# Causal masks added into the key bias by GpSimd, two runs of score products joined, and an order of transposes and copies to go with it

## The chip, the cores and the metric

The kernel runs on one core of a Trainium2 chip (trn2). The metric is the time of one execution on the device in microseconds (us), lower is better. The kernel before took 1081.54 us, the median of 3 runs (1081.49 to 1081.89).

## What is computed

Three layers in a row: causal attention with a decay bias, a mixture of 8 experts, and a product of two linear maps. Only the attention matters for the change:

```python
def _attn_ref(q, k, v, s):              # q, k, v: (2, 8, 576, 64); s: (2, 8, 576)
    scores = scale * np.matmul(q, k.transpose(0, 1, 3, 2))
    causal = np.triu(np.ones((S, S), dtype=bool), k=1)
    cum = np.cumsum(np.maximum(s, 0.0), axis=-1)
    bias = -(cum[:, :, :, None] - cum[:, :, None, :])
    scores = np.where(causal, -1000000000.0, scores + np.minimum(bias, 0.0))
    scores = scores - np.max(scores, axis=-1, keepdims=True)
    attn = np.exp(scores)
    attn = attn / (np.sum(attn, axis=-1, keepdims=True) + 1e-09)
    return np.matmul(attn, v)
```

Behind it come x @ w1[e], a ReLU and @ w2[e] for the experts, weighted by a gate of 8 Sinkhorn rounds, and (x @ w_a) * (x @ w_b) @ w_out. All is fp32 on the outside; the kernel splits fp32 numbers into a high and a low fp32r part and makes three products of each.

## The kernel before, in words

The attention takes the first 10% of the time. Its 16 heads go in 8 pairs. A loop over k from -1 to 8, written out by hand on each engine, is a software pipeline: in period k the scores of pair k are made while the probabilities of pair k-1 are transposed and multiplied with v, and pair k-2 is scaled into x. S_k below is the moment at which TensorE begins period k, with the tail transposes of pair k (line 1626). Within one pair, 576 query tokens are four tiles of 128 (t = 0 to 3) and a tail of 64 of both heads; tile t needs keys 0 to 128(t+1).

The order of TensorE in a period (lines 1813 to 1840): transpose_qk(k, 2), score(k, 0) with tiles 0 and 1, transpose_p(k-1, 5), the masks of tiles 0 and 1, transpose_p 2, score(k, 1) with tile 2, transpose_p 7, mask of tile 2, transpose_p 1, transpose_qk(k+1, 0), transpose_p 4, transpose_qk(k+1, 1), score(k, 2) with tile 3, transpose_p 3, mask, transpose_p 6, score_tail(k, 0), transpose_p 0, score_tail(k, 1) with its mask, spread_recips(k-1, 1) and (k-1, 0), attend(k-1, 1) and (k-1, 0). The score products (line 1662) use 64 rows of the array for each head, two heads side by side; all else uses 128 rows. A causal mask is a bf16 product of an identity with a triangle of large negative numbers, added into the same PSUM bank (lines 1671 and 1706): 8 of 128 columns and 1 of 64 for each pair.

VectorE adds the key bias to the scores while it reads them from PSUM and keeps the row minimum (biased, line 1179, biased_tail, line 1194; semaphore sc_done, 10 steps a pair), splits q and k (low_qk, 1157, 1160), copies some of the transposed probabilities out of PSUM (copy_pT, 1220), and makes the reciprocals of the row sums (invert, 1212). ScalarE makes the exponentials (exp_tile, 820; exp_tail, 830) and the other copies (798). The transposed probabilities go through a ring of two PSUM banks, so each transpose_p waits until the unit two places before it was copied.

GpSimd in period k (lines 706 to 724): spread_tail_queries(k) (630), wide_reciprocals(k-1) (641 and 644; TensorE's spread_recips(k-1) waits for them on rec_wide), low_x(k-2) (653), and in some periods work on the first expert weights.

The key bias is a row of cumulative sums, broadcast by DMA from DRAM to 128 partitions. SyncE issues all these loads in one queue, in program order. load_bias(p) (line 517) waits for sc_done of the tail of pair p-2, then issues two loads of 256 KB (line 523) and two of 144 KB for the tail (line 526); load_v and load_qk follow. In the kernel before only VectorE waits for them, at the first biased of pair p.

## Time and profile before

| | |
|---|---|
| median of 3 runs | 1081.54 us (1081.49 to 1081.89) |
| profiled execution | 1081.88 us, of which its span is 1080.1 us |
| TensorE busy | 1073.8 us (99%) |
| VectorE, ScalarE, GpSimd busy | 705.0, 425.4, 336.7 us |
| mean granted TensorE clock | 0.998 |

The page of the profile covers the whole program; the attention is its first 97 us. The span runs from the first to the last instruction; the execution's own time has 1.8 us around it. A group of instructions is told by its line, engine, operation and the tiles it writes and reads. "Idle before, <- releaser" is how long the engine had stood still before an instruction and what let it go. TensorE's matmuls are pipelined: their durations overlap, so the distance from one start to the next is the cost of one.

### The profile page before, as it was taken

What the parts mean: (1) busy time and instruction counts of PE and PEld (TensorE: products, weight loads), DVE (VectorE), ACT (ScalarE), POOL (GpSimd) and SP (SyncE); (2) the same over time, 40 slices, a digit from 0 to 9 for tenths busy, and PEclk for the clock granted to TensorE, in tenths of its full rate; (3) what the DMA queues carried; (4) which work ended last, traced back from release to release, by engine and by line L of the source; (5) the groups of instructions that cost most, each with busy time, mean ns of one, the idle gap of its engine ahead of it and who ended that gap; (6) DMA issues with size and microseconds to landing.
All of it is one profiled execution on the core that took longest, in us unless ns stands there. A gap on an engine that the chain in (4) does not pass through costs nothing.

```text
span 1080.1 us, 19243 instructions
## 1 busy us (share of the span) xinstructions
PE 1073.8 (99%) x6746; PEld 969.3 (90%) x6746; DVE 705.0 (65%) x1497; ACT 425.4 (39%) x984; POOL 336.7 (31%) x441
## 2 busy tenths in 40 slices
PE   9999999999999999999999999999999999999999
PEld 7777989899898998989899898989989899898997
DVE  7778966566574666657566564756656697586682
ACT  6888637143241523325152341614234433132230
POOL 1446604132140412214041231404223375144420
PEclk9999999999999999999999999999999999999999
DMA  8862111101111111121111111111212002102002
GB/s 184 196 141 71 59 40 40 56 26 57 59 39 39 39 58 37 41 58 39 39 39 58 39 45 52 39 39 39 59 40 59 21 21 79 40 21 77 22 1 88
DMA packets 91702, 59.27 MB, mean 55 GB/s; under 512 B 32736, under 2 KB 78048, under 8 KB 91648
## 3 DMA queue, kind: packets, MB, share of 16 engines
q1 hardware_dynamic: 90416, 58.23, 19.1%
q8 instruction: 32, 0.52, 0.2%
q10 hardware_dynamic: 1232, 0.33, 0.2%
q14 instruction: 22, 0.18, 0.1%
HBM read 56.15 MB, written 2.40 MB: 54 GB/s over the span
## 4 chain that ended last, share of the span: by engine, by line
PE 98%; DVE 1%; ACT 1%; issue 0%; POOL 0%; DVEq 0%
PE bank L1783 15%; PE bank L1785 15%; PE bank L1784 15%; PE bank L1912 14%; PE bank L1914 14%; PE bank L1913 14%; PE bank L1731 2%; PE bank L1768 2%; PE bank L1662 2%; PE bank L1618 1%; PE bank L1702 0%; PE bank L1809 0%; PE bank L1791 0%; DVE kept_c L1264 0%; PE bank L1743 0%; PE bank L1942 0%
## 5 line engine op out<-in xcount | busy, mean ns | idle before, releaser
L701 POOL TENSOR_TENSOR hl<-kept_c,hh 128x320 fp32r<-128x320 f32 (+1 forms) x128 | 104.9, 820 | 525.1 <-ACT kept_c L901 525.1
L1912 PE MATMUL bank<-w2h,hh 128*128 128x512 f32 x680 | 266.6, 392 | 0.0
L1914 PE MATMUL bank<-w2h,hl 128*128 128x512 f32 x680 | 265.1, 390 | 0.0
L1913 PE MATMUL bank<-w2l,hh 128*128 128x512 f32 x680 | 265.1, 390 | 0.0
L1432 DVE SCALAR_TENSOR_TENSOR acc<-bank,P,acc 128x512 f32<-128x512 f32 x135 | 101.3, 751 | 196.1 <-PE bank L1914 196.1
L1783 PE MATMUL bank<-xh,w1h 128*128 128x320 f32 (+1 forms) x704 | 210.1, 298 | 1.0 <-DVE kept_c L1264 0.9
L1264 DVE TENSOR_TENSOR kept_c<-bank,kept_c 128x256 f32<-128x256 f32 (+1 forms) x440 | 183.8, 453 | 38.3 <-PE bank L1785 34.9
L1785 PE MATMUL bank<-xh,w1l 128*128 128x320 f32 (+1 forms) x704 | 208.7, 296 | 0.0
L1784 PE MATMUL bank<-xl,w1h 128*128 128x320 f32 (+1 forms) x704 | 208.6, 296 | 0.0
L899 ACT ACTIVATE hh<-kept_c 128x256 fp32r<-128x256 f32 (+1 forms) x256 | 113.1, 443 | 155.7 <-DVE kept_c L1264 155.7
L798 ACT ACTIVATE kept_one<-bank 128x256 f32<-128x256 f32 (+1 forms) x88 | 34.8, 395 | 322.7 <-PE bank L1785 322.6
L1783 PE MATMUL bank<-th,w1h 128*128 128x320 f32 (+1 forms) x528 | 156.9, 297 | 0.1
L1784 PE MATMUL bank<-tl,w1h 128*128 128x320 f32 (+1 forms) x528 | 156.5, 296 | 0.0
L1785 PE MATMUL bank<-th,w1l 128*128 128x320 f32 (+1 forms) x528 | 156.5, 296 | 0.0
L1914 PEld LDWEIGHTS bank<-w2h,hl 128*128 128x128 f32 x680 | 127.7, 188 | 26.9
L1912 PEld LDWEIGHTS bank<-w2h,hh 128*128 128x128 f32 x680 | 127.8, 188 | 25.4
L1913 PEld LDWEIGHTS bank<-w2l,hh 128*128 128x128 f32 x680 | 127.8, 188 | 25.3
L1783 PEld LDWEIGHTS bank<-xh,w1h 128*128 128x128 f32 x704 | 133.7, 190 | 3.7 <-DVE kept_c L1264 2.7
L1784 PEld LDWEIGHTS bank<-xl,w1h 128*128 128x128 f32 x704 | 133.7, 190 | 0.7
L1785 PEld LDWEIGHTS bank<-xh,w1l 128*128 128x128 f32 x704 | 133.6, 190 | 0.0
L1264 DVE TENSOR_TENSOR kept_c<-bank,kept_one 128x320 f32<-128x320 f32 (+1 forms) x176 | 75.9, 455 | 40.8 <-PE bank L1785 30.0
L1783 PEld LDWEIGHTS bank<-th,w1h 128*128 128x128 f32 x528 | 100.3, 190 | 0.4 <-ACT kept_one L798 0.3
(155 smaller groups left out, 1420.7 us busy)
## 6 DMA issues: line engine op xcount, KB each, us to landing
raw<-in_moe_w SPq DMA_DIRECT2D x32, 512.0 KB, 3.6
raw<-in_moe_w SPq DMA_DIRECT2D x32, 256.0 KB, 2.7
raw<-in_moe_w SPq DMA_DIRECT2D x64, 128.0 KB, 2.7
bias<-cum_dram SPq DMA_DIRECT2D x14, 256.0 KB, 3.6
raw<-in_moe_w_a SPq DMA_DIRECT2D x12, 256.0 KB, 2.9
raw<-in_moe_w_b SPq DMA_DIRECT2D x24, 128.0 KB, 2.9
raw<-in_moe_w_out SPq DMA_DIRECT2D x6, 512.0 KB, 3.9
bias_tail<-cum_dram SPq DMA_DIRECT2D x16, 144.0 KB, 4.2
```

The lines of the kernel that those rows point to most:

```text
L701: pool.tensor_tensor(hl[:, 3 - place, columns(b, s)], src[:, 0:width(s)], hh[:, place, columns(b, s)].bitcast(F32), ALU.subtract).then_inc ...
L798: return act.activation(out_, in_, ACT.Copy).then_inc(sem_, 1)
L899: act.activation(hh[:, m % 2 + 2 * half, columns(b, s)], src[:, 0:width(s)], ACT.Relu).then_inc(h_hi, 1)
L1264: dve.tensor_tensor(to[:, 0:width(s)], product_bank(nth, n, first)[:, 0:width(s)], other[:, 0:width(s)], ALU.add).then_inc(done, 1)
L1432: dve.scalar_tensor_tensor(out=acc[:, tile, :], in0=bank[:, :], scalar=P[:, tile, bass.ds(e, 1)], in1=acc[:, tile, :], op0=ALU.mult, op1=A ...
L1662: pe.matmul(S_BANK[first + r][:, col:col + n], qk[z][rows, a, 0, t * PART:(t + 1) * PART], qk[z][rows, b, 1, 0:n], start=(nth == 0 and i = ...
L1783: pe.matmul(bank, high, right(n, False, c, s), start=(c == 0), stop=False)
L1784: pe.matmul(bank, high, right(n, True, c, s), start=False, stop=False)
L1785: ins = pe.matmul(bank, low, right(n, False, c, s), start=False, stop=(c == 1))
L1912: pe.matmul(bank, hh[:, place, at], w2h[:, place, :], start=(nth == 0), stop=False)
L1913: pe.matmul(bank, hh[:, place, at], w2l[:, place, :], start=False, stop=False)
L1914: ins = pe.matmul(bank, hl[:, 3 - place, at], w2h[:, place, :], start=False, stop=(nth == 3))
```

## The change

It works on pairs 1 to 7; pair 0 keeps its mask products, because its bias rows come through PSUM. Each bias tile becomes eight blocks of 128 keys. SyncE loads the four blocks of keys into places 2 to 5 and, in one more load for each head (64 KB), the first block into place 0. The new GpSimd function mask_bias(p) waits for all six loads of pair p and writes masked copies: place 1 (keys 0), 7 (keys 1), 6 (keys 2), and place 5 (keys 3) in place, then the tail's 64 columns. A tile of queries then reads its blocks with a stride: places 1; 2 and 7; 0, 3 and 6; 2 to 5. VectorE's first biased of a pair waits for bias_masked instead of bias_loaded. mask_bias(k+1) stands between spread_tail_queries(k) and wide_reciprocals(k-1) in GpSimd's order. On TensorE score(k, 1) follows score(k, 0) at once, and the transposes behind them change places; VectorE moves copy_pT(5) and add_eps back, ScalarE moves exp_tile(k, 0, 0) and high_qk(k+1, 0) forward and high_x back. The bias of odd pairs moves to the room of the last features of x.

```diff
--- before.py
+++ after.py
@@ -60,6 +60,7 @@
     FC = FE // PART
     GC = 4
     GROUPS = FP // PART // GC
+    BIAS_BLOCKS = 8
 
 
     PARTS = [(0, SPLIT), (SPLIT, S)]
@@ -141,21 +142,34 @@
 
 
 
-    qk, nat, bias, bd, bias_tail, scores, scores_tail, vt, spread = ([None] * 2 for _ in range(9))
+    qk, nat, bd, bias_tail, scores, scores_tail, vt, spread = ([None] * 2 for _ in range(8))
     qk[0], at = sb("qk_0", [PART, 2, 2, S], F32R, slot_at[1])
     nat[0], at = sb("nat_0", [PART, 2, QT, 2, D], F32, at)
     assert at <= slot_at[1] + 2 * 7 * 2 * PART * 4
     qk[1], at = sb("qk_1", [PART, 2, 2, S], F32R, th_end - 2 * 2 * S * 4)
     assert at <= th_end
     at = tl_end - 2 * 2 * S * 4
-    for z in range(2):
-        bias[z], at = sb(f"bias_{z}", [PART, 2, MAIN], F32, at)
+
+
+    bias_0, at = sb("bias_0", [PART, 2, BIAS_BLOCKS * PART], F32, at)
     bd[0], at = sb("bd_0", [PART, 2, PART], F32R, at)
     assert at <= tl_end
     at = hh_at
     for z in range(2):
         bias_tail[z], at = sb(f"bias_tail_{z}", [PART, S], F32, at)
     assert at <= hh_at + N * 4
+
+    last_features = (B * KC - 2) * S * 4
+    bias_1 = [sb("bias_1_0", [PART, BIAS_BLOCKS * PART], F32, 16512 + last_features)[0],
+              sb("bias_1_1", [PART, BIAS_BLOCKS * PART], F32, 16512 + B * KC * S * 4 + last_features)[0]]
+    assert BIAS_BLOCKS * PART <= 2 * S
+
+    def bias_of(z, r):
+        return bias_0[:, r, :] if z == 0 else bias_1[r][:, :]
+
+    def bias_blocks(z, r):
+        return bias_of(z, r).rearrange("p (n s) -> p n s", s=PART)
+
 
     pT_at = at
     pT, at = sb("pT", [PART, 2, QT, S], F32, at)
@@ -222,6 +236,7 @@
     k_loaded = [sem(f"k_loaded{z}") for z in range(2)]
     first_tails = sem("first_tails")
     v_loaded = [sem(f"v_loaded{z}") for z in range(2)]
+    bias_masked = sem("bias_masked")
     bias_loaded = [sem(f"bias_loaded{z}") for z in range(2)]
     w1_loaded = [sem(f"w1_loaded{i}") for i in range(2)]
     w2_loaded = [sem(f"w2_loaded{i}") for i in range(2)]
@@ -411,6 +426,15 @@
 
 
 
+    FIRST_KEYS = 2 * PART
+    TILE_BLOCKS = [slice(1, 2), slice(2, 8, 5), slice(0, 7, 3), slice(2, 6)]
+
+    def loads_of_bias(p):
+
+        return 6 * (p // 2 + 1) - (4 if p % 2 == 0 else 0)
+
+
+
     UNIT_NTH = {5: 1, 2: 2, 7: 3, 1: 4, 4: 5, 3: 6, 6: 7, 0: 8}
     BY_DVE = {5: 1, 4: 2, 3: 3}
     BY_ACT = {2: 1, 7: 2, 1: 3, 6: 4, 0: 5}
@@ -520,8 +544,11 @@
                 sp.wait_ge(sc_done, 10 * (p - 2) + 10)
             if p > 0:
                 for r in range(2):
-                    sp.dma_start(bias[z][:, r, :],
-                                 cum_ap[2 * p + r:2 * p + r + 1, 0:MAIN].broadcast_to([PART, MAIN])).then_inc(bias_loaded[z], DMA)
+                    row = cum_ap[2 * p + r:2 * p + r + 1, :]
+                    sp.dma_start(bias_of(z, r)[:, FIRST_KEYS:FIRST_KEYS + MAIN],
+                                 row[:, 0:MAIN].broadcast_to([PART, MAIN])).then_inc(bias_loaded[z], DMA)
+                    sp.dma_start(bias_of(z, r)[:, 0:PART],
+                                 row[:, 0:PART].broadcast_to([PART, PART])).then_inc(bias_loaded[z], DMA)
             for r in range(2):
                 sp.dma_start(bias_tail[z][r * TAIL:(r + 1) * TAIL, :],
                              cum_ap[2 * p + r:2 * p + r + 1, :].broadcast_to([TAIL, S])).then_inc(bias_loaded[z], DMA)
@@ -644,6 +671,22 @@
             pool.tensor_scalar(tail_recips[:, :], tail_ident[:, :], recips[:, p % 2, TAIL_COLUMN:TAIL_COLUMN + 1], None,
                                ALU.mult).then_inc(rec_wide, 1)
 
+        def mask_bias(p):
+
+            if not (present(p) and p > 0):
+                return
+            z = p % 2
+            pool.wait_ge(bias_loaded[z], DMA * loads_of_bias(p))
+            mask = maskb[:, :].rearrange("p (o s) -> p o s", o=1)
+            for r in range(2):
+                blocks = bias_blocks(z, r)
+                pool.tensor_tensor(blocks[:, 1:8:6, :], blocks[:, 2:4, :], mask.broadcast_to([PART, 2, PART]), ALU.add)
+                pool.tensor_tensor(blocks[:, 6, :], blocks[:, 4, :], maskb[:, :], ALU.add)
+                ins = pool.tensor_tensor(blocks[:, 5, :], blocks[:, 5, :], maskb[:, :], ALU.add)
+            ins.then_inc(bias_masked, 1)
+            pool.tensor_tensor(bias_tail[z][:, MAIN:S], bias_tail[z][:, MAIN:S], maskt[:, :],
+                               ALU.add).then_inc(bias_masked, 1)
+
         def low_x(p, g):
             if not 0 <= p < PAIRS - 1:
                 return
@@ -705,6 +748,7 @@
         pool.wait_ge(const_set, 6)
         for k in PERIODS:
             spread_tail_queries(k)
+            mask_bias(k + 1)
             wide_reciprocals(k - 1)
             low_x(k - 2, 0)
             low_x(k - 2, 1)
@@ -864,7 +908,7 @@
         def first_bias_rows():
             for half in range(2):
                 act.wait_ge(first_bias_mm, half + 1)
-                copy(bias[0][:, :, half * SPLIT:(half + 1) * SPLIT],
+                copy(bias_0[:, :, FIRST_KEYS + half * SPLIT:FIRST_KEYS + (half + 1) * SPLIT],
                      FIRST_BIAS[half][:, :].rearrange("p (r s) -> p r s", r=2), first_bias)
 
         def high_t(i, c, s=None):
@@ -925,15 +969,15 @@
             high_qk(k, 2)
             exp_tile(k - 1, 2, 1)
             exp_tail(k - 1)
+            exp_tile(k, 0, 0)
             copy_pT(k - 1, 2)
+            high_qk(k + 1, 0)
             copy_pT(k - 1, 7)
-            exp_tile(k, 0, 0)
-            high_qk(k + 1, 0)
             copy_pT(k - 1, 1)
-            high_x(k - 2, 0)
             high_qk(k + 1, 1)
             if k == -1:
                 first_bias_rows()
+            high_x(k - 2, 0)
             exp_tile(k, 1, 0)
             high_x(k - 2, 1)
             copy_pT(k - 1, 6)
@@ -1175,9 +1219,11 @@
                 dve.wait_ge(first_bias, 1 if t < 2 else 2)
             elif (t, r) == (0, 1):
                 at_least(dve, pt_mm, 8 * (p - 1))
-                dve.wait_ge(bias_loaded[z], DMA * (4 * (p // 2 + 1) - (2 if z == 0 else 0)))
-            dve.tensor_tensor_reduce(scores[z][:, r, COL[t]:COL[t + 1]], bank[:, col:col + n], bias[z][:, r, 0:n],
-                                     -1.0 / INV, 3.0e38, ALU.add, ALU.min, neg_max[:, z, c:c + 1]).then_inc(sc_done, 1)
+                dve.wait_ge(bias_masked, 2 * p)
+            blocks = slice(2, 2 + t + 1) if p == 0 else TILE_BLOCKS[t]
+            dve.tensor_tensor_reduce(scores[z][:, r, COL[t]:COL[t + 1]].rearrange("p (n s) -> p n s", s=PART),
+                                     bank[:, col:col + n].rearrange("p (n s) -> p n s", s=PART),
+                                     bias_blocks(z, r)[:, blocks, :], -1.0 / INV, 3.0e38, ALU.add, ALU.min, neg_max[:, z, c:c + 1]).then_inc(sc_done, 1)
 
         def biased_tail(p, half):
             if not present(p):
@@ -1325,12 +1371,12 @@
             scale_x(k - 2, 0)
             low_qk(k, 2)
             scale_x(k - 2, 1)
-            copy_pT(k - 1, 5)
             biased(k, 0, 1)
             biased(k, 0, 0)
+            biased(k, 1, 1)
+            copy_pT(k - 1, 5)
+            biased(k, 1, 0)
             add_eps(k - 1)
-            biased(k, 1, 1)
-            biased(k, 1, 0)
             biased(k, 2, 0)
             copy_pT(k - 1, 4)
             biased(k, 2, 1)
@@ -1659,11 +1705,14 @@
                 for i, (a, b) in enumerate(TERMS):
                     for r in range(2):
                         rows = slice(r * D, (r + 1) * D)
-                        pe.matmul(S_BANK[first + r][:, col:col + n], qk[z][rows, a, 0, t * PART:(t + 1) * PART],
-                                  qk[z][rows, b, 1, 0:n], start=(nth == 0 and i == 0), stop=False)
+                        ins = pe.matmul(S_BANK[first + r][:, col:col + n], qk[z][rows, a, 0, t * PART:(t + 1) * PART],
+                                        qk[z][rows, b, 1, 0:n], start=(nth == 0 and i == 0),
+                                        stop=(p > 0 and nth == len(tiles) - 1 and i == 2))
+            if p > 0:
+                ins.then_inc(sc_mm, 1)
 
         def score_masks(p, g):
-            if not present(p):
+            if p != 0:
                 return
             first, tiles = SCORE_TILES[g]
             for nth, (t, col) in enumerate(tiles):
@@ -1701,8 +1750,8 @@
             for i, (a, b) in enumerate(TERMS):
                 ins = pe.matmul(S_BANK[2 + half][:, 0:HALF], bd[z][:, a, :],
                                 qk[z][:, b, 1, half * HALF:(half + 1) * HALF], start=(i == 0),
-                                stop=(i == 2 and half == 0))
-            if half == 1:
+                                stop=(i == 2 and (half == 0 or p > 0)))
+            if half == 1 and p == 0:
                 ins = pe.matmul(S_BANK[3][:, MAIN - HALF:HALF], identb[:, :], maskt[:, :], start=False, stop=True)
             ins.then_inc(sc_mm, 1)
 
@@ -1813,16 +1862,16 @@
         for k in range(-1, PAIRS):
             transpose_qk(k, 2)
             score(k, 0)
+            score(k, 1)
+            score_masks(k, 0)
+            score_masks(k, 1)
             transpose_p(k - 1, 5)
-            score_masks(k, 0)
             transpose_p(k - 1, 2)
-            score(k, 1)
+            transpose_qk(k + 1, 0)
             transpose_p(k - 1, 7)
-            score_masks(k, 1)
             transpose_p(k - 1, 1)
-            transpose_qk(k + 1, 0)
+            transpose_qk(k + 1, 1)
             transpose_p(k - 1, 4)
-            transpose_qk(k + 1, 1)
             if k == -1:
                 spread_first_bias()
             score(k, 2)
```

## Rows read from the trace of the kernel before

**Rows 1.** The page, busy time of each engine over the whole span.

```profile
PE 1073.8 (99%) x6746; PEld 969.3 (90%) x6746; DVE 705.0 (65%) x1497; ACT 425.4 (39%) x984; POOL 336.7 (31%) x441
```

**Rows 2.** Busy by stretch: us, PE, PEld, DVE, ACT, POOL, clock, DMA share, GB/s.

```profile
50.80:62.27 11.47, 11.47 (x110) 8.97 (x109) 8.84 (x31) 10.07 (x32) 5.37 (x8) 1.00 0.58 151
...
9.85:13.26 3.41, 3.41 (x20) 2.71 (x19) 2.33 (x13) 0.97 (x3) 0.73 (x1) 0.50 0.64 200
```

**Rows 3.** Timeline of PE, periods 2 and 4: start, us, line, op, tiles, count.

```profile
27.86 0.28 PE L1626 MATMUL bank<-ident,nat 64*128 64x64 f32 x1
...
50.80 0.27 PE L1626 MATMUL bank<-ident,nat 64*128 64x64 f32 x1
...
52.30 0.39 PE L1671 MATMUL bank<-maskb,identb 128*128 128x128 bf16 x4
52.52 0.50 PE L1731 MATMUL bank<-ident,scores 128*128 128x128 f32 x3
52.95 0.79 PE L1662 MATMUL bank<-qk 64*128 64x384 f32 x6
53.67 0.33 PE L1731 MATMUL bank<-ident,scores_tail 128*128 128x128 f32 x1
53.83 0.28 PE L1671 MATMUL bank<-maskb,identb 128*128 128x128 bf16 x2
53.95 0.61 PE L1731 MATMUL bank<-ident,scores 128*128 128x128 f32 x4
54.39 0.60 PE L1618 MATMUL bank<-ident,nat 128*128 128x128 f32 x4
...
55.79 0.96 PE L1662 MATMUL bank<-qk 64*128 64x512 f32 x6
56.68 0.55 PE L1731 MATMUL bank<-ident,scores 128*128 128x128 f32 x3
...
58.63 0.20 PE L1706 MATMUL bank<-maskt,identb 128*128 128x64 bf16 x1
58.67 0.41 PE L1743 MATMUL bank<-ident,wide_recips 128*128 128x128 f32 x2
...
62.27 0.27 PE L1626 MATMUL bank<-ident,nat 64*128 64x64 f32 x1
```

**Rows 4.** Timeline of SyncE's queue: loads of bias for pairs 1, 2 and 5.

```profile
11.23 1.09 SPq L526 DMA_DIRECT2D bias_tail<-cum_dram  x2
...
17.14 0.81 SPq L523 DMA_DIRECT2D bias<-cum_dram  x2
...
49.85 0.81 SPq L523 DMA_DIRECT2D bias<-cum_dram  x2
51.10 1.10 SPq L526 DMA_DIRECT2D bias_tail<-cum_dram  x2
```

**Rows 5.** Tile bias_tail on SyncE's queue: issue to landing, all sixteen loads.

```profile
DMA to landing us min/median/max: 3.2/4.2/5.6
```

**Rows 6.** Timeline of POOL: period 4, and the rest of a later one.

```profile
51.86 0.73 POOL L630 TENSOR_TENSOR bd<-qk,own_half 128x256 fp32r<-128x256 f32 x1 [2.19 <-DVE qk L1160]
56.82 0.61 POOL L641 COPY wide_recips<-recips 128x512 f32<-128x512 f32 x1 [4.23 <-DVE recips L1212]
57.41 0.44 POOL L644 TENSOR_SCALAR tail_recips<-tail_ident,recips 128x64 f32<-128x64 f32 x1
...
95.18 1.41 POOL L660 TENSOR_TENSOR tl<-xr,th 128x576 fp32r<-128x576 f32 x1
```

**Rows 7.** Timeline of DVE: pair 1's first biased, last copy and end of period 4.

```profile
18.50 0.28 DVE L1179 CUSTOM_DVE_ANT_0 scores<-bank,bias 128x128 f32<-128x128 f32 x1
...
57.27 0.56 DVE L1220 COPY pT<-bank 128x384 f32<-128x384 f32 x1 [0.52 <-PE bank L1731]
...
61.20 0.08 DVE L1194 DVE_READ_ACCUMULATOR2_ANT neg_max<- 128x1 f32 x1
```

## The prediction

> **What bounds the kernel now.** I read the page first: TensorE is busy 1073.8 us of the 1080.1 us span [rows 1], so whatever shortens its stream shortens the kernel, and whatever makes it wait lengthens it. Next the busy time by stretch over one period of the attention, S_4 = 50.80 to S_5 = 62.27: TensorE has no idle time in 11.47 us, ScalarE works 10.07, VectorE 8.84, GpSimd 5.37 [rows 2]. Periods 2 to 6 repeat this, so with S_2 = 27.86 [rows 3] S_3 is about 39.3 and S_7 about 85.2. Then the timelines of the other engines inside that period, to see how late each may be before TensorE feels it. GpSimd's wide_reciprocals(3) ran from 56.82 to 57.85 [rows 6], and TensorE took them up at 58.67 [rows 3]: 0.8 us to spare. Ahead of them GpSimd stood idle 4.23 us, waiting for VectorE's reciprocals [rows 6]. That hole is where mask_bias goes. Last the loads of bias: those of pair 5 were issued from 49.85 on [rows 4], 0.95 us before S_4, right after the tail of pair 3 was biased. The last of them, the second of the two tail loads at 51.10 [rows 4], was issued at about 51.6; with the median of 4.2 us to landing [rows 5] it is there at 55.8, or S_4 + 5.0.
>
> **What TensorE saves.** Cost is read from start to start [rows 3]. Four masks: 52.30 to 52.52, 0.22 us. Two masks: 53.83 to 53.95, 0.12, and the two behind tile 3 the same. The tail's: 58.63 to 58.67, 0.04. Together 0.50 us a period. Joining score(k, 0) and score(k, 1) saves one change between 64-row and 128-row work. Six products of 384 columns take 52.95 to 53.67, 0.72; six of 512 take 55.79 to 56.68, 0.89 [rows 3]. The three steps in which two heads run side by side thus cost 0.17 more for 128 columns more, so 0.51 for 384, and 0.21 is not columns. The three transposes ahead take 0.43 (52.52 to 52.95) where four take 0.44 (53.95 to 54.39), so 0.10 too much, and the first transpose behind takes 0.16 instead of 0.11. 0.21 + 0.10 + 0.05 = 0.36 us go with one change. Sum: 0.86 us a period, 11.47 to 10.61, if nothing else makes TensorE wait; over periods 1 to 7 it is 6.0 us. Pair 0 keeps its masks; its VectorE chain, not TensorE, sets the start of period 1, so nothing is counted there.
>
> **The new order of transposes and copies** costs nothing by itself. Laid out from the same distances, score(k, 1) ends at S + 1.5, transposes 5, 2, the first of q and k, then 7 start at S + 1.5, 2.0, 2.3, 2.8. Unit 7 needs VectorE's copy of unit 5, now behind three biased calls; these start at about S + 1.4 and the copy ends at S + 2.8, so 0.1 us of wait at most. ScalarE's copies of units 2 and 7 come just in time by the same count. Its 10.07 us of work [rows 2] fit into 10.61. VectorE's strided reads cover the same elements; I count 0, and 0.1 us a call as the upper end, which its idle time would cover in most places. VectorE waited 0.52 us for transpose 3 before the copy at 57.27, and from there on ran without a gap to the last minimum of the tail at 61.28, S + 10.5 [rows 7]. Transpose 3 comes 0.86 earlier, so the tail is biased at S + 9.7 (bounds 9.6 and 10.5).
>
> **What mask_bias adds.** SyncE's queue gets two more loads for each pair, ahead of the tail loads. A load of bias takes 0.4 us to issue (two in 0.81 [rows 4]), so the last tail load goes out 0.8 us later. From the first issue to the last landing it was 1.8 + 4.2 = 6.0 in period 4, and with the slowest landing, 5.6 [rows 5], 7.4. With 0.8 on top, 6.8 to 8.2; I take 7.0, nearer to the median, and 5.9 as the low end (nothing lost by the added loads). They delay load_v and load_qk by the same 0.8 us, which land a period before they are used.
>
> The masks themselves are seven GpSimd instructions: for each head one of 256 elements and two of 128, and one of 64. Such an instruction on 256 elements took 0.73 us, on 576 1.41 [rows 6], so 2.1 ns an element and 0.19 fixed: 0.73, 0.46, 0.46, twice, and 0.33 is 3.63, and as neighbours overlap by some 0.04 (57.41 against 56.82 + 0.61), 3.4 us. Low end 2.3, the elements alone; high end 5.1, each as dear as the one of 256. VectorE and GpSimd ran side by side when the 0.73 was taken. The Trainium skill (GPSIMD Engine Reference, Specifications) says the two share an SBUF interface and collide when a VectorE instruction has two SBUF inputs or runs in a two-port mode. By that rule the masks keep their 3.4 us, because VectorE takes one operand from PSUM in nearly everything it does in that stretch; if those collided too, it would be nearer to 5.1.
>
> **Where it lands.** mask_bias(k+1) waits for loads which come S_k + 5 or later, and wide_reciprocals(k-1), then low_x(k-2), stand behind it in GpSimd's order. TensorE's spread_recips(k-1) waits for them, and attend and the whole next period stand behind that. So there is a chain from the biased tail of pair k-1 to the start of period k+1: loads 7.0, masks 3.4, reciprocals 1.03 (56.82 to 57.85), then TensorE's 3.60 from 58.67 to 62.27 [rows 3]. That is 15.03. In the old timetable, with the tail of pair 3 at 49.85, GpSimd would be ready at 61.3, not 57.85. Write E_k for the biased tail, S_k + 9.7: S_(k+1) = E_(k-1) + 15.03 = S_(k-1) + 24.73. So two periods last 24.73, 12.4 each, against 11.47 before. It is not worse because a late period gives the next loads a head start.
>
> The start: the loads of pair 2 go out at 17.14 [rows 4], right after E_0. S_2 = 17.14 + 15.03 = 32.2, not 27.86. In period 1 VectorE also waits: the last load for pair 1, issued at about 11.7 [rows 4], is there at 11.7 + 4.2 + 0.8 = 16.7, its masks at 20.1, and the first biased of pair 1, at 18.50 before [rows 7], could be at 17.9 without the copy ahead of it. Three biased calls and the copy of unit 5 let transpose 7 go at 21.7, 2.8 us late. E_1, 26.9 before (1.0 ahead of S_2, as 61.28 of S_5), is then 26.9 - 0.8 + 2.8 = 28.9. From there S_3 = 28.9 + 15.03 = 43.9, S_4 = 32.2 + 24.73 = 56.9, S_5 = 68.7, S_6 = 81.7, S_7 = 93.4; the last is 8.2 later than 85.2. None lies below the 10.61 us that TensorE needs. In period 7 no masks are made and TensorE gains again; GpSimd's tail reciprocals come late there already, so I count 0.5 of the 0.86. What follows is bound by TensorE and shifts whole. Sum: +8.2 - 0.5 = +7.7 us on the profiled execution's 1081.88, so 1089.6; that execution was 0.34 above the median of the runs, and so I write 1089.2.
>
> All low ends together (9.6 + 5.9 + 2.3 + 1.03 + 3.6 = 22.4 for two periods, S_2 at 29.9) give 2.1 - 5 x 0.25 - 0.5, about +0.3: 1082. All high ends (10.5 + 8.2 + 5.1 + 1.03 + 3.6 = 28.4, S_2 at 35.1) give 7.2 + 5 x 2.7 - 0.5, +20: 1102, which would need them all at once.
>
> **Rivals.** (a) The masks are hidden, TensorE keeps its gain: 1081.54 - 6.0 = 1075.5. It needs the last landing by about S + 2.5, so that 3.4 + 1.03 end at S + 7.0, where TensorE now wants the reciprocals. Against it stands S + 5.0 [rows 4, 5]; for it, only that I misjudge GpSimd's order, or that loads start earlier than I see. If ScalarE's 10.07 us and its waits turn out to be the bound, 2 or 3 us of the 6 go, still faster. Chance 0.11.
> (b) The clock falls. In the stretch 9.85 to 13.26 the granted clock was 0.50, that is 1.2 GHz, after a start of thin products and waits; TensorE has full work elsewhere and 1.00 [rows 2]. My timetable makes it idle 1 to 2.5 us in each of six periods, nearly 5 in period 1. One such stretch loses 1.7 us of work; two to five of them on top of the forecast give 1093 to 1098, say 1095. The decision point is whether an idle stretch at the spread of reciprocals is followed by a clock of 0.50. The Trainium skill (TensorE: Matmul & The Clock Gate, Why this matters for your kernels) warns of idle gaps between bursts of matmuls; by it period 1 is the likeliest to be hit and the short gaps are not. Chance 0.17.
> (c) Wash: the chain is near its low ends, TensorE's saving and the waits cancel: 1082. Chance 0.06.
> (d) The change does not do what it says, as when the masks stay on TensorE: the diff leaves no mask for p > 0, so under 0.01.
> Forecast: 0.66.
>
> **Numbers.** About 0.2% can be told from no change here. Slower: forecast, (b), and a part of (c), 0.83; same 0.05; faster 0.12. The range reaches from the low ends to the clock rival, 1082 to 1099.
>
> **What the changed profile would show.** GpSimd: wide_reciprocals straight behind the masks, waiting for a DMA before the masks, seven instructions of 3.4 us together. TensorE: idle before line 1743's transposes, released by GpSimd's tail_recips, in turns 1.1 and 2.4 us, no bf16 products from pair 1 on, periods in turns of 11.7 and 13.0. VectorE: an idle stretch of 2 us before the first biased of pair 1, released by GpSimd. The forecast is wrong if TensorE's periods are near 10.6 (then (a)), or if the granted clock falls (then (b)), or if the masks take much less than 3 us or the last bias load lands before S + 4.

## The result, and the profile after

The changed kernel took **1099.72 us** (median of 4 runs, 1098.37 to 1100.85) against 1081.72 for the kernel before on the same chip: a ratio of 1.0169, 95% interval [1.0157, 1.0182], or 18.0 us slower. The forecast was 1089.2, with a range of 1082 to 1099. The profiled execution took 1098.37 us, 16.5 more than the profiled one of before, and the rows below explain these 16.5.

The page of the changed kernel: span, then busy time of each engine. It answers to [rows 1].

```profile
span 1096.6 us, 19180 instructions
...
PE 1075.1 (98%) x6683; PEld 967.8 (88%) x6683; DVE 705.4 (64%) x1497; ACT 425.6 (39%) x984; POOL 358.0 (33%) x490
```

TensorE has 63 products fewer and yet a span 16.5 us longer. GpSimd has 49 instructions more, seven for each of seven pairs, and 21.3 us more work. That is 3.04 us a pair.

S_k, the start of period k, read in the timeline of TensorE at the tail transposes of each pair, for the kernel before, the forecast and the changed kernel:

| | S_1 | S_2 | S_3 | S_4 | S_5 | S_6 | S_7 |
|---|---|---|---|---|---|---|---|
| before | 15.43 | 27.86 | 39.34 | 50.80 | 62.27 | 73.74 | 85.22 |
| forecast | | 32.2 | 43.9 | 56.9 | 68.7 | 81.7 | 93.4 |
| after | 14.98 | 35.12 | 47.74 | 62.53 | 73.95 | 89.80 | 101.66 |

At S_7 the changed kernel is 16.4 us behind; the last attend product starts 16.5 later (124.43 against 107.89), and nothing is added or won back after that. The loss lies in periods 1 to 6. From period 2 on the periods are shorter and longer in turn, as forecast, but the loss is twice the size (the forecast had 8.2 at S_7).

Waits in the first 120 us of the changed kernel: engine, tile and line waiting, what for, total us, times, longest.

```profile
POOL bias L683 <- DMA bias_tail<-cum_dram: 28.3, 7, 8.2
...
PE bank L1792 <- POOL tail_recips L671: 10.9, 7, 3.2
```

The first is new; of the second the kernel before had 0.7 us, once. GpSimd stands in front of the masks until the last tail load is there, and TensorE stands in front of spread_recips (L1792) until GpSimd gets to the reciprocals behind the masks. The same in the timeline of GpSimd in period 4; it answers to [rows 6]:

```profile
66.12 0.67 POOL L683 TENSOR_TENSOR bias<-bias,maskb 128x256 f32<-128x256 f32 x1 [1.80 <-DMA bias_tail<-cum_dram]
66.76 0.42 POOL L684 TENSOR_TENSOR bias<-bias,maskb 128x128 f32<-128x128 f32 x1
...
68.93 0.31 POOL L687 TENSOR_TENSOR bias_tail<-bias_tail,maskt 128x64 f32<-128x64 f32 x1
69.17 0.61 POOL L668 COPY wide_recips<-recips 128x512 f32<-128x512 f32 x1
69.77 0.44 POOL L671 TENSOR_SCALAR tail_recips<-tail_ident,recips 128x64 f32<-128x64 f32 x1
```

TensorE at the end of period 3 and in period 4; it answers to [rows 3]. In brackets, the idle time before the instruction and what ended it.

```profile
57.42 0.66 PE L1792 MATMUL bank<-ident,wide_recips 128*128 128x128 f32 x2 [2.19 <-POOL tail_recips L671]
...
58.76 3.85 PE L1817 MATMUL bank<-pT,vt 128*64 128x320 f32 x28
62.53 0.27 PE L1672 MATMUL bank<-ident,nat 64*128 64x64 f32 x1
...
62.68 1.46 PE L1708 MATMUL bank<-qk 64*128 64x128 f32 x17
64.06 0.98 PE L1780 MATMUL bank<-ident,scores 128*128 128x128 f32 x7
64.88 0.60 PE L1664 MATMUL bank<-ident,nat 128*128 128x128 f32 x4
...
70.36 0.41 PE L1792 MATMUL bank<-ident,wide_recips 128*128 128x128 f32 x2 [0.34 <-POOL tail_recips L671]
...
71.09 2.93 PE L1817 MATMUL bank<-pT,vt 128*64 128x320 f32 x28
73.95 0.28 PE L1672 MATMUL bank<-ident,nat 64*128 64x64 f32 x1
```

No bf16 product is left in these periods, and the score products of tiles 0 to 2 stand together. The seven waits for tail_recips are 2.05, 1.54, 2.19, 0.34, 3.20, 0.79 and 0.82 us. The first attend takes 3.85 us and the second 2.93: the first fell into a stretch of half clock. Busy time by stretch, columns as in [rows 2]:

```profile
57.24:60.65 3.41, 3.23 (x14) 2.04 (x16) 0.53 (x2) 1.79 (x7) 3.30 (x5) 0.50 0.86 207
84.55:87.96 3.41, 3.32 (x14) 2.04 (x16) 0.00 (x0) 1.88 (x7) 3.41 (x5) 0.50 0.40 122
```

There is one more such stretch, in period 1, where the kernel before had the full clock. TensorE had waited 3.21 us there for VectorE, which itself waited for the masks of pair 1:

```profile
23.58 0.48 PE L1780 MATMUL bank<-ident,scores_tail 128*128 128x128 f32 x1 [3.21 <-DVE pT L1266]
...
26.55 0.96 PE L1708 MATMUL bank<-qk 64*128 64x512 f32 x6
```

```profile
23.12:26.52 3.40, 2.94 (x13) 2.64 (x13) 1.30 (x6) 2.45 (x6) 0.00 (x0) 0.50 0.85 208
```

VectorE before the first biased of pair 1, and SyncE's queue for pair 5; they answer to [rows 7] and [rows 4]:

```profile
22.07 0.29 DVE L1224 CUSTOM_DVE_ANT_0 scores<-bank,bias 128x128 f32<-128x128 f32 x1 [4.53 <-POOL bias_tail L687]
```

```profile
57.83 0.34 SPq L548 DMA_DIRECT2D bias<-cum_dram  x1
58.21 0.43 SPq L550 DMA_DIRECT2D bias<-cum_dram  x1
58.68 0.43 SPq L548 DMA_DIRECT2D bias<-cum_dram  x1
59.16 0.43 SPq L550 DMA_DIRECT2D bias<-cum_dram  x1
59.63 1.12 SPq L553 DMA_DIRECT2D bias_tail<-cum_dram  x2
```

The forecast had these loads down from the first issue to the last landing in 7.0 us. Here the masks begin 8.29 us after the first issue (66.12 - 57.83); for pairs 2 to 7 it is 8.8, 7.8, 8.0, 8.3, 7.8 and 9.8.

### The profile page after: what moved, and what is told of

It reads as the page before. It is cut to its first block, busy times and chain, and to the rows that moved or that the text cites. A ratio compares the mean times of both kernels' runs of the same rounds, so it can differ in the third digit from the quotient of the medians.

```text
span 1096.6 us, 19180 instructions
## 1 busy us (share of the span) xinstructions
PE 1075.1 (98%) x6683; PEld 967.8 (88%) x6683; DVE 705.4 (64%) x1497; ACT 425.6 (39%) x984; POOL 358.0 (33%) x490
## 4 chain that ended last, share of the span: by engine, by line
PE 91%; POOL 3%; issue 2%; SPq 2%; DVE 1%; ACT 1%; DMA 1%; DVEq 0%; POOLq 0%; ACTq 0%
PE bank L1832 15%; PE bank L1834 15%; PE bank L1833 14%; PE bank L1961 14%; PE bank L1963 14%; PE bank L1962 14%; PE bank L1817 2%; POOL bias L683 1%; DVE kept_c L1310 1%; DMA bias_tail<-cum_dram 1%; PE bank L1792 1%; SPq L530 0%; PE bank L1780 0%; POOL bias L684 0%; POOL bias L685 0%
```

## The experiments

Each kernel is the changed one with the edit shown, and was timed in five rounds beside the kernel before.

### 1. Only the order in GpSimd's queue

```diff
             spread_tail_queries(k)
-            mask_bias(k + 1)
             wide_reciprocals(k - 1)
+            mask_bias(k + 1)
```

> The changed kernel with mask_bias(k+1) put behind wide_reciprocals(k-1) on GpSimd, nothing else. Theory (the place in GpSimd's queue costs the time): the reciprocals are there before TensorE wants them, its idle time at the spread of reciprocals is gone, periods 2 to 7 take 10.6 us each, 0.86 less than in the kernel before, 5.2 in all. The wait of VectorE for the masks of pair 1 stays, so S_2 is near 32 instead of 27.9, about 4.1 lost. Sum 1081.7 - 5.2 + 4.1 = 1080.6 us (1079 to 1082.5). Rival (the order of transposes and copies, or VectorE's strided reads, cost the time): periods stay above 12 us and the time above 1090.

**Measured:** 1085.92 us (1083.72 to 1086.85), ratio 1.0037 [1.0024, 1.0051], above the expected range. The two lines exchanged are worth 13.8 us of the 18.0. Of the 10.9 us for which TensorE waited for tail_recips, 0.8 are left (from 20 to 113 us, grouped by line):

```profile
L1792 PE MATMUL bank<-ident,wide_recips 128*128 128x128 f32 x32 | 6.2, 275 | 0.8 <-POOL tail_recips L671 0.8
```

Most periods are 10.90 us, 0.57 below those of before. The queue order is the mechanism. That it stays 4.2 us above before instead of just below has two places: S_2 is 32.94, since VectorE still waits for pair 1's masks (4.41 us, and TensorE behind it meets half the clock from 23.2 to 26.8 as in the changed kernel), and period 5 is 12.35.

### 2. Pair 1 keeps its masks on TensorE as well

```diff
-            if not (present(p) and p > 0):
+            if not (present(p) and p > 1):
                 return
```

(With it, pair 1 has four loads, TensorE's masks for p in (0, 1), and VectorE waits for the loads of pair 1.) The order of experiment 1 stays.

> As the run before it, and the masks of pair 1 stay on TensorE as those of pair 0 do, so VectorE waits for the loads of pair 1 alone, which are four again. Theory: S_2 is near 27.5, 0.36 earlier than in the kernel before (the joined products), and periods 2 to 7 take 10.6 us: 1081.7 - 5.2 - 0.36 = 1076.2 us (1075 to 1077.5). Rival (something else in the start costs it, such as the new order at pair 0): the same as the run before it, 1080 or more.

**Measured:** 1081.95 us, ratio 1.0005 [0.9996, 1.0014]; 1076.2 was expected. By the medians pair 1 was 4.0 us of what was left. S_2 is back at 27.21, but the profiled execution also has no half clock near 10 us, and its S_1, 13.48, is 1.6 earlier than in experiment 1. Period 5 is still 12.43, and its waits (59.0 to 72.3) are:

```profile
POOL bias L684 <- DMA bias_tail<-cum_dram: 5.0, 2, 3.6
DVE scores L1228 <- POOL bias_tail L688: 1.6, 1, 1.6
```

The masks of pair 5 are late for VectorE. In SyncE's queue its bias loads (from 50.96) stand behind three loads of expert weights (from 49.26), which may be why; experiments 7 and 8 try it.

### 3. The clock: work for TensorE while it waits

```diff
+            if part == 1:
+                for _ in range({0: 34, 1: 26, 2: 37, 4: 55}.get(p, 0)):
+                    pe.matmul(bank[:, 0:PART], identb[:, :], maskb[:, :], start=True, stop=True)
             pe.wait_ge(rec_wide, 2 * p + 2)
```

> The changed kernel with bf16 products without use (34, 26, 37 and 55, at some 0.056 us each) ahead of the wait for the reciprocals of pairs 0, 1, 2 and 4, so that TensorE works through the idle time of periods 1, 2, 3 and 5. Theory (the later of the two chains sets the time, and the two stretches of half clock at 57 and 85 us lie on the other): the granted clock stays at 1.00 after 27 us, attend of periods 3 and 5 is 1.5 us shorter, and the time moves by less than 1 us, 1098.7 to 1100.2. Rival (the half clock adds to the end): 2 x 1.5 us less, 1096.7 us or lower.

**Measured:** 1099.95 us (1097.64 to 1100.29), the same as the changed kernel. TensorE's idle time for tail_recips at the spread fell from 10.9 to 5.4 us, and the two stretches of half clock at 57.2 and 84.6 are gone. But the clock did not stay at 1.00, as was expected: period 1 keeps its stretch (24.2 to 27.8), and a new one begins at 72.1. It falls into period 4, whose end is S_5, and the way from the spread to S_5 takes 5.22 us instead of 3.6. In this kernel's profiled execution S_7 is 103.42, 1.8 later than in the changed one. So the equal times alone do not say what the two stretches cost.

The changed kernel's own trace says more. Its two stretches lengthened periods 3 and 5 by 1.5 us each (5.1 from the spread to the next period, 3.6 at full clock). Yet at the next spread TensorE still waited, 0.34 and 0.79 us, for reciprocals whose chain had begun with bias loads issued at 57.83 and 84.03, when the tails of pairs 3 and 5 were biased. Pairs 3, 5 and 7 hang on that chain of their own, from tail to loads to masks to reciprocals, and it arrives last at S_5 and S_7. Without these two stretches TensorE would have waited there longer instead. The stretch of period 1 is another matter: it lies ahead of the tail of pair 1, with which that chain begins.

### 4. The joined products and the new order, without the masks' move

All masks stay on TensorE, no loads are added, mask_bias does nothing.

```diff
         def score_masks(p, g):
-            if p != 0:
+            if not present(p):
                 return
```

> The joined products and the order of transposes and copies alone: all masks on TensorE, two loads of bias for each head pair and two of the tail as in the kernel before, VectorE waits for the loads. Theory: 0.36 us less in each of 7 periods, 1081.7 - 2.5 = 1079.2 us (1078.5 to 1080). Rival (the new order makes TensorE wait for copies and gives the gain back or more): 1081.7 us or above.

**Measured:** 1082.5 us, ratio 1.0008 [0.9999, 1.0017]; periods of 11.53 us, where 11.47 - 0.36 = 11.11 was the forecast. The rival's value came. TensorE in period 4:

```profile
52.22 0.51 PE L1718 MATMUL bank<-maskb,identb 128*128 128x128 bf16 x6
52.57 0.93 PE L1778 MATMUL bank<-ident,scores 128*128 128x128 f32 x7
53.34 0.60 PE L1662 MATMUL bank<-ident,nat 128*128 128x128 f32 x4
54.17 0.33 PE L1778 MATMUL bank<-ident,scores_tail 128*128 128x128 f32 x1 [0.23 <-DVE pT L1264]
```

Four transposes cost 0.44 [rows 3], so unit 7's, due at 53.78, begins 0.39 late: it needs the bank of unit 5. The gain of joining goes into a wait for the ring of two banks.

### 5 and 6. Is it VectorE's order, or the place of transpose 7?

Experiment 4 with VectorE's copy of unit 5 moved forward:

```diff
             biased(k, 0, 0)
-            biased(k, 1, 1)
             copy_pT(k - 1, 5)
+            biased(k, 1, 1)
```

> Run e4 (joined products and new order, all masks on TensorE) with the copy of unit 5 ahead of biased(k, 1, 1). Theory (the joined products are worth 0.36 us a period, and the late copy gave them back: transpose 7 waited some 0.4 us in e4): periods of 11.53 go to 11.2, 2.3 us less than e4: 1080.2 us. Rival (joining is worth nothing): as e4, 1082.5.

**Measured:** 1081.38 us, ratio 1.0000 [0.9991, 1.0008], periods 11.37, where 11.2 was expected. Experiment 4 with transpose 7 behind both transposes of q and k:

```diff
             transpose_qk(k + 1, 0)
+            transpose_qk(k + 1, 1)
             transpose_p(k - 1, 7)
             transpose_p(k - 1, 1)
-            transpose_qk(k + 1, 1)
```

> Run e4 (joined products and new order, all masks on TensorE) with transpose 7 moved behind both transposes of q and k. Theory: the ring wait that gave the gain of the joined products back is gone, 0.36 us less in each of 7 periods than in the kernel before: 1079.2 us, periods of 11.1. Rival (joined products are worth no more than 0.1): 1081 or more, periods above 11.35.

**Measured:** 1081.07 us, 0.9999 [0.9990, 1.0008], periods 11.25, where 11.1 and 1079.2 us were expected. The place of the transpose helps more than the place of the copy: with the copy forward, transpose 5 starts at 52.16, VectorE copies it at 52.80 to 53.49, and transpose 7, ready at 53.37, still begins 0.18 late.

```profile
52.16 0.93 PE L1778 MATMUL bank<-ident,scores 128*128 128x128 f32 x7
52.93 0.60 PE L1662 MATMUL bank<-ident,nat 128*128 128x128 f32 x4
53.55 0.33 PE L1778 MATMUL bank<-ident,scores_tail 128*128 128x128 f32 x1
```

```profile
52.80 0.69 DVE L1264 COPY pT<-bank 128x512 f32<-128x512 f32 x1
```

Of the 0.36 forecast for joining, 0.22 is reached in the best order tried, and -0.06 in the change's own. Neither shows in the time of the whole kernel. In the best order S_7 is 1.2 us earlier than before, and the last attend starts only 0.6 earlier (104.57 against 105.19); where the rest goes was not followed.

### 7 and 8. Two tries at period 5

Experiment 2 with VectorE's copy forward, and that again with two of the expert weights' loads issued behind the bias and v loads of the same period:

```diff
-            if p in (1, 3):
-                load_unit(p // 2, p // 2, w1f[0, :, :, 0, p // 2, :], w1f[0, :, :, 1, p // 2, :])
...
                 load_v(p + 1)
+            if p in (1, 3):
+                load_unit(p // 2, p // 2, w1f[0, :, :, 0, p // 2, :], w1f[0, :, :, 1, p // 2, :])
```

> Run e2 with VectorE's copy of unit 5 one biased call earlier, ahead of biased(k, 1, 1). Theory (behind three biased calls the copy holds transpose 7 by 0.18 us and a restart, so the periods are 10.90 instead of 10.61): periods of 10.6 to 10.7 where nothing else waits, 0.2 to 0.3 less in each of 7, 1.5 to 2 us less than e2, so 1080.2 us. The extra 1.5 us in period 5 (VectorE waits for masks whose loads went out late) stays. Rival (the 0.29 is the changed products themselves): as e2.

> As e5, and SyncE issues the expert weights of pairs 1 and 3 behind the loads of bias and v instead of ahead of them. Theory: the loads of bias for pair 5 go out 2 us earlier, the wait of VectorE for their masks and the 1.5 us of period 5 are gone, 1.5 us less than e5: 1078.7 us. Rival (the queue is full anyway, so the loads land as late): as e5.

**Measured:** 1083.18 us, 1.0016 [1.0007, 1.0025], and 1082.92 us, 1.0009 [0.9998, 1.0020]. Both missed. The undisturbed periods are 11.06 and 10.90 us, so an earlier copy gains nothing over experiment 2 (10.90). In the first, periods 4 and 5 are 12.4 and 14.6, the latter with half the clock from 66.4 on. With the weights later, periods 4 to 6 are 12.1, 11.7 and 11.6, where experiment 2 had 10.9, 12.4 and 10.9. The bias loads of pair 5 went out at 50.98, no earlier than the 50.96 of experiment 2 (0.5 us earlier counted from S_4), where 2 us were expected, so what delays them is not settled by this: the wait only moved.

### 9. The changed kernel without its two added loads

Tile 2 reads plain blocks and loses its causal mask with them.

```diff
-    TILE_BLOCKS = [slice(1, 2), slice(2, 8, 5), slice(0, 7, 3), slice(2, 6)]
+    TILE_BLOCKS = [slice(1, 2), slice(2, 8, 5), slice(2, 5), slice(2, 6)]
...
-                    sp.dma_start(bias_of(z, r)[:, 0:PART],
-                                 row[:, 0:PART].broadcast_to([PART, PART])).then_inc(bias_loaded[z], DMA)
```

> The changed kernel without the two added loads of 64 KB for each pair: tile 2 reads places 2 to 4, so the causal mask of tile 2 is left out, and mask_bias waits for four loads. The seven masks and their place in GpSimd's queue stay. Theory (from the first issue to the last landing the changed kernel takes 7.7 to 9.8 us where the kernel before took 5.7 to 7.0, and the chain of two periods holds this time whole): the loads take 1.3 us less, six such times in two chains, so three in the one that ends last and one at the start: 4 us less than the changed kernel, 1095.7 us (1094 to 1097.5). Rival (the loads land late because of the other traffic, not because of the added ones): less than 1 us, 1099.

**Measured:** 1089.43 us (1087.36 to 1090.10), ratio 1.0067 [1.0054, 1.0080], 10.3 us below the changed kernel, where 4 were expected, with GpSimd's order as bad as before. The masks now begin 6.6, 7.7, 5.7, 6.4, 5.9 and 7.2 us after the first issue, 6.6 on average where the changed kernel had 8.4. TensorE's idle time at the spread is 8.3 us:

```profile
L1790 PE MATMUL bank<-ident,wide_recips 128*128 128x128 f32 x30 | 6.4, 299 | 8.3 <-POOL tail_recips L669 8.3
```

S_7 comes at 93.38, 8.3 us ahead of the changed kernel's (the profiled execution here was the slowest of its five, and the changed kernel's the fastest of its four). These are also the forecast's S_7 (93.4) and its time (1089.2). That is luck: this kernel lacks the loads that the forecast had counted at 0.8 us a pair.

### 10. The added loads in number, but tiny

As in experiment 9, tile 2 reads plain blocks and goes without its causal mask, and nothing reads the tiny loads.

```diff
-                    sp.dma_start(bias_of(z, r)[:, 0:PART],
-                                 row[:, 0:PART].broadcast_to([PART, PART])).then_inc(bias_loaded[z], DMA)
+                    sp.dma_start(bias_of(z, r)[0:1, 0:PART],
+                                 row[:, 0:PART]).then_inc(bias_loaded[z], DMA)
```

> The changed kernel with its two added loads for each pair kept in number and place, but cut from 128 rows of 512 B to one row of 512 B; nobody reads them, and tile 2 is left without its causal mask, as in e9. So the queue has the same number of issues as the changed kernel and hardly more bytes or rows than e9. Two theories of the 10.3 us that the added loads cost. (1) Their number costs: each issue and each completion is a fixed price in front of the tail loads; then about 1096 to 1099 us, and the time from first issue to last landing stays near 7.7 to 9.7 us. (2) Their rows cost: the 128 row descriptors written at the issue and carried by the queues; then about 1089 to 1091 us, 5.6 to 7.6 us to the last landing as in e9, and two issues close together take less than the 0.4 us each of the full loads. I think (2) has two thirds of the chance.

**Measured:** 1088.08 us (1087.72 to 1089.61), ratio 1.0065 [1.0051, 1.0079]. Two issues more for each pair cost nothing that can be measured; the masks begin 6.0 us after the first issue on average. So it is not the number of loads, but what they carry. The queue, for pair 5:

```profile
53.12 0.34 SPq L548 DMA_DIRECT2D bias<-cum_dram  x1
53.50 0.29 SPq L550 DMA_DIRECT2D bias<-cum_dram  x1
...
54.55 1.12 SPq L553 DMA_DIRECT2D bias_tail<-cum_dram  x2
```

From the first issue to the first tail load it is 1.43 us, against 1.80 in the changed kernel: the issue explains 0.4 of the 2.4 us between the two (8.4 and 6.0). The rest lies between the issue and the landing. Busy time from 3.0 us after the first issue until the masks begin, in the changed kernel (pair 4) and in this one (pair 5; the columns before the last are the clock and the DMA engines' busy share):

```profile
48.20:53.11 4.91, 4.89 (x45) 3.91 (x43) 3.81 (x17) 4.71 (x14) 0.92 (x2) 1.00 0.95 225
```

```profile
56.00:59.18 3.18, 3.16 (x26) 2.75 (x28) 2.23 (x11) 2.98 (x10) 0.14 (x1) 1.00 0.96 234
```

In these two stretches all 16 DMA engines are busy nearly to the landing of the last tail load. They are of different pairs, though, and by their GB/s the first moved 0.36 MB more, where the added loads are 0.13 MB; so they do not give the price. Taken over pairs 2 to 7, from the first issue to the masks, the busy share times the length is 6.3 us of all engines a pair in the changed kernel, 4.8 in experiment 9 and 4.3 here, with 1.42, 1.28 and 1.17 MB moved. So by this estimate the two loads of 128 rows cost 1.5 to 2.0 us of all engines, some of it other traffic that falls into the longer wait. Whether the 256 rows or the 128 KB set that price was not tried. Pair 7 of the changed kernel, with 9.8 us the longest, has a busy share of only 0.63, and for it this does not account.

### 11 and 12. Put together

Masks behind the reciprocals, pair 1 on TensorE, transpose 7 behind both transposes of q and k, and GpSimd copies the first block instead of a load:

```diff
+                pool.tensor_copy(blocks[:, 0, :], blocks[:, 2, :])
                 pool.tensor_tensor(blocks[:, 1:8:6, :], blocks[:, 2:4, :], mask.broadcast_to([PART, 2, PART]), ALU.add)
```

> Run e2 (masks behind the reciprocals, pair 1 on TensorE) with the first block copied by GpSimd (two instructions of 128 elements, some 0.3 us each) instead of two added loads, and transpose 7 of the probabilities moved behind both transposes of q and k. Theory: two things ate the gain of e2: the added loads, which fill SyncE's queue so that the masks of pair 5 come 1.6 us late, and the ring (transpose 7 starts 0.77 us behind unit 5's last transpose and must wait for its 0.69 us copy, 0.24 lost a period). Both gone, the periods 2 to 7 are 10.6 us: 1081.7 - 0.36 - 6 x 0.86 = 1076.2 us (1075 to 1077.5). Rival (the loads and the ring are not it): 1080.5 to 1082 as e2.

**Measured:** 1079.01 us (1078.55 to 1080.35) against 1081.04 for the kernel before (27 runs), ratio 0.9982 [0.9973, 0.9991]. It beats both kernels, by 2.0 and by 20.7 us, though 1076.2 was expected. The page:

```profile
PE 1069.7 (99%) x6692; PEld 965.6 (90%) x6692; DVE 707.6 (66%) x1497; ACT 425.6 (40%) x984; POOL 357.7 (33%) x495
```

Periods 2 to 5 are 10.80 us each, where before had 11.47, and period 6 is 11.18. With the weights' loads moved as well:

> Run e10 with the expert weights of pairs 1 and 3 issued behind the loads of bias and v. Theory: with the added loads gone SyncE is ahead of its waits, so this changes nothing, within 0.5 us of e10. Rival (the queue still makes the masks of pairs 3 and 5 late): e10 shows a wait of VectorE for masks in period 3 or 5 and this run is 0.5 to 1.5 us faster.

**Measured:** 1079.36 us, 0.9982 [0.9973, 0.9991], periods 2 to 5 again 10.80: no difference, as expected. Without the added loads no period is longer for the place of the weights' loads.

## Why the prediction was right in kind and wrong in size

The direction, the place and the rhythm were right; the time, 1099.72, lies above the range, which ended at 1099, though below the sum of all high ends, 1102. What the runs said of each step:

**The chain** (masks in front of the reciprocals in GpSimd's order) is shown by experiment 1: 13.8 us go with two exchanged lines, and the waits that go with them are those which the changed kernel's own profile shows. Rival (a), masks hidden, falls.

**The step that failed** is the term "loads 7.0" of the chain, and in it the sentence "with 0.8 on top". I priced the two added loads at the time that SyncE needs to issue them, and left out the time to carry them. In the kernel before, the DMA engines' busy share (the column before the last) in the stretch in which pair 5's bias loads land was this:

```profile
52.80:55.80 3.00, 3.00 (x30) 2.43 (x27) 2.38 (x13) 1.93 (x7) 0.00 (x0) 1.00 0.87 227
```

At 0.87 there is little room, so whatever is put in ahead of the tail loads can delay them by its own transfer. Measured, the loads took 8.4 us to the start of the masks, above the forecast's high end of 8.2, and 6.6 without the added ones: 1.9 each pair, not 0.8. Pair 7 took 9.8.

How this adds up to S_7, which hangs on three such links, one behind the other (pairs 3, 5, 7), and on the tail of pair 1 ahead of them. Against the forecast the changed kernel's S_7 is 8.3 us late. The three links took 7.83, 8.29 and 9.81 us instead of 7.0 each, 4.9 more. The tail of pair 1 was biased at 32.08 instead of 28.9, 3.2 more. The tails of pairs 3 and 5 came 0.4 later after their periods' start than forecast (below), 0.8 together, and TensorE's last part took 3.74 instead of 3.60, 0.4 in three links. The masks gave 1.0 back.

The same for the changed kernel against experiment 9, 8.3 us at S_7. The three links took 7.65, 6.36 and 7.15 us there, so the added loads made 4.8 in them. The tail of pair 1 was biased at 28.21, 3.9 earlier. Of these, 2.5 are that pair 1's last load landed at 16.27 instead of 18.77. The other 1.4 are the half clock of period 1: from transpose 7 to the score products of tile 3 the changed kernel took 2.97 us (23.58 to 26.55, above), experiment 9 1.57 at full clock:

```profile
21.11 0.33 PE L1778 MATMUL bank<-ident,scores_tail 128*128 128x128 f32 x1 [1.75 <-DVE pT L1264]
...
22.68 0.96 PE L1706 MATMUL bank<-qk 64*128 64x512 f32 x6
```

From there to the biased tail both took the same 5.5 us. The sum is 8.7, and 0.4 of it does not reach S_7, since in experiment 9 TensorE's own work and not GpSimd set S_3.

That experiment 9 met the forecast's 1089.2 does not mean that all else in it was right. The forecast had counted the added loads four times on the way to S_7, 3.2 us; without them it would have been 3.2 lower, at 90.2. So of its error of 8.3 us at S_7, 5.1 is the price of the added loads, with the clock that came with their lateness, and 3.2 is the rest, most of it the loads' time without them: 6.2 forecast, 7.1 on average measured in these three links.

**A smaller miss in the same direction:** the tail of pair k was biased at S_k + 10.1, not 9.7. SyncE's next bias loads go out at 45.20, 57.83, 72.61 and 84.03, all 10.1 after S_2 to S_5. VectorE won half of the 0.8 us that I gave it. Transpose 7's wait for the ring is part of it (it starts at 65.50, four transposes after 64.88, so 0.18 late); the rest was not followed.

**The masks** took 3.05 us, forecast 3.4, bounds 2.3 and 5.1. Instructions of the masks over the attention, min/median/max in ns:

```profile
L683 POOL TENSOR_TENSOR bias<-bias,maskb x14: 667/672/682, 18.8 to 95.2; 128x256 f32<-128x256 f32 x14
L684 POOL TENSOR_TENSOR bias<-bias,maskb x14: 422/428/435, 19.5 to 95.9; 128x128 f32<-128x128 f32 x14
```

Pair 1's (from 18.84) ran while VectorE stood still for the 4.53 us before 22.07, the others beside its work, and all took the same within 15 ns. The Trainium skill (GPSIMD Engine Reference, Specifications) has GpSimd contend with VectorE instructions that have two SBUF inputs or run in a two-port mode. The trace agrees in so far as VectorE's two-input instructions beside the masks of pairs 4 and 5 (biased, low_qk) had one operand in PSUM, and the masks were no slower.

**TensorE's saving.** The masks were forecast at 0.50 us a period. Pairs of kernels with the same order on TensorE and VectorE that differ in them (and in GpSimd's masks and the loads) give 11.53 to 10.90 (experiments 4 and 2), 11.37 to 11.06 or 10.90 (5 and 7 or 8) and 11.25 to 10.80 (6 and 11): 0.63, 0.31 or 0.47, and 0.45. Joining was forecast at 0.36 with "0.1 us of wait at most"; in the change's own order the wait ate it all (11.53 against 11.47), and the best order got 0.22. In the changed kernel neither counted, as TensorE had over 10 us of waits.

**The clock.** Rival (b)'s condition came true, and with it one of the prediction's own signs of being wrong. Two waits at the spread, 2.19 and 3.20 us, were met with 0.50, others of 2.05 and 1.54 were not; and in period 1 the wait of 3.21 us for VectorE was met with 0.50 too. Its price came true in part. The two stretches at the spread lay on the chain that had time to spare, by the changed kernel's trace; the one of period 1 lay on the chain that ended last and cost 1.4 us at S_7. No experiment took it away by itself, so these 1.4 us rest on the comparison of the two traces. The Trainium skill (TensorE: Matmul & The Clock Gate, Why this matters for your kernels) warns of long idle gaps between bursts of matmuls. The forecast took from it that period 1 was the likeliest to be hit and the short gaps were not; period 1 was hit, but so was TensorE after 2.19 us, and there the trace does not agree. The resulting time (1099.7) lies nearer to rival (b)'s 1095 than to the forecast, mostly for another reason: of the 10.5 us above the forecast the clock's known part is 1.4. Rival (c), the wash, would have needed the chain at its low ends, and (d) is refuted by the 63 products that are gone.

## What to carry to other kernels

An added load costs its issue and also its transfer, and here, where the DMA engines were busy already, the second was the larger part: look at their share in the stretch before the landing that is waited for, not at the mean. Before work is put into a hole of an in-order engine, ask what the hole was waiting for and what stands behind it; here moving the new work one place back was worth 13.8 us. Leaving the added loads out was worth 10.3 with GpSimd's order unchanged; copying the 64 KB on chip in their place was tried only together with the moved transpose (experiment 11), some 2.5 us below experiment 2 by the ratios. A wait of TensorE can cost more than its length: here the clock was halved behind waits of 2.19, 3.20 and 3.21 us, though not behind 1.54 and 2.05, so look at the granted clock behind every long wait of the chain that ends last. A gain on the bounding engine shows only if the ring of buffers behind it lets the engine go faster, so try the order without the rest of the change.

## What was not expected of the hardware

- A stretch of half clock at about 10 us, 3.41 us long, is there in some executions and not in others of nearly the same program: experiment 11 has it from 9.31 and S_1 at 14.92, experiment 12, which differs only in later loads of weights, has none there and S_1 at 13.43. What decides it is open. The changed kernel, the kernel before and experiments 1, 3, 4, 5, 6, 8 and 9 have it too, experiments 2, 7 and 10 do not.
- Two broadcast loads of 64 KB, 128 rows of 512 B each, cost all 16 DMA engines some 1.5 to 2.0 us by the estimate of experiment 10, when two loads of a single row at the same place in the queue cost nothing that can be measured (1088.08 against 1089.43 us without them).
- VectorE's strided reads of the blocks cost nothing: its sum is 705.4 us, 705.0 before.
